# Clearing the region tails earlier and transposing a block ahead in an attention + mixture-of-experts + feed-forward kernel

## Chip, cores and metric

The kernel runs on one NeuronCore of a Trainium2 chip. The metric is the device time of one launch in microseconds (us), the median of several runs. Engines are TensorE (PE in the profile, PEld for its weight loads), VectorE (DVE), ScalarE (ACT), GpSimd (POOL) and SyncE (SP). SP issues most of the DMAs; a row with a q behind the engine's name (SPq, ACTq) is work of that engine's instruction sequencer: a register load, a branch, the issue of a DMA.

## What is computed

Three stages follow one another on 3072 tokens (4 sequences of 768) of width 384, all in float32.

```
for t in range(S):                                   # 1: gated linear attention, complex decay
    S_re, S_im = (ar*S_re - ai*S_im + k[t] (x) v[t], ar*S_im + ai*S_re)
    y[t] = q[t] . S_re
...
e_idx = argmax(x @ w_gate, axis=1)                   # 2: top-1 mixture of 8 experts
for e in range(E):
    mask = e_idx == e
    h = np.maximum(x[mask] @ w1[e], 0.0)
    out[mask] = gate_w[mask, None] * eom[mask, e, None] * (h @ w2[e])
...
h = x @ w_in                                         # 3: leaky feed-forward
return np.maximum(0.01 * h, h) @ w_out
```

## The kernel before

**Attention** (0 to about 290 us) works on 24 chunks of 128 tokens. Each finished row, its gate and its token number go from an SBUF ring to a DRAM table `x_sorted` (in the code `xs`): the table has one region per expert, and POOL scatters 128 rows of 386 floats with one indirect DMA (`scatter`, L563). The last two scatters belong to the last group of chunks.

**Tails.** The last block of a region is read as a full 128 rows, so the 128 rows behind each region's end must be zero. They are written from a constant tile `zeros`, one DMA of 128 x 386 floats per expert, as soon as DVE has written the ends (`ends_i`, semaphore `s_ends`). SP clears the tails of experts 0 and 1 (L1834 to L1837) and ACT those of experts 2 to 7 (L1997 to L2001). ACT does so only when the first block's tokens have landed (`s_xb`), and ahead of its first `relu`.

**The unused path.** Between attention and the expert stage DVE, ACT and PE each load a flag (L1352) and jump over a general attention path that these inputs don't need (the branches are L1389 on ACT, L1506 on DVE, L1601 on PE). After its jump ACT increments `s_moved` (L169), for which SP waits before it loads the first block.

**Experts** (about 293 to 569 us) work on blocks of 128 sorted rows, 29 of them here. The steps of block g:

- `load(g)` on SP: four DMAs that bring the block to the single buffer `x_q`, when `turn_tokens(g-1)` has emptied it (`s_tx`); `gates(g)`: one small DMA of the gates; `store(g)`: the block's result to `y_sorted`, when `result(g)` has made it. SP runs them in the order `load(g+3)`, `gates(g+2)`, `store(g)`.
- `turn_tokens(g)` on DVE: a 32 x 32 transpose from `x_q` to the PSUM bank `tx_bank` (L2025). `block_tokens(g)` on DVE: two instructions that split the bank into a leading and a trailing part in `x_tr` (L2031, L2033), when layer 1 of the block before is done with `x_tr`.
- `layer1(g)` on PE: 18 matmuls. `relu(g)` on ACT: two. `transpose_hidden(g)` on PE: 8. `leading(g)` on ACT and `trailing(g)` on DVE: two each, making `h_tr`. `layer2(g)` on PE: 24 matmuls. `result(g)` on DVE: one copy to `y_b` (L2046), when `store(g-1)` has landed.

PE runs `transpose_hidden(g)`, `layer1(g+1)`, `layer2(g)` in a loop over g. All instructions of an engine run in the order in which they are written; semaphores tie the engines together. Before block 0 DVE works out the table of blocks in small dependent steps: the first part (`s_rows`) gives the rows of each block, the second (`s_table`) the rest. PE fills its wait there with dummy transposes (`keep_warm`, L2203): 40, a wait on `s_rows`, then 22 more.

POOL meanwhile splits the next expert's weights (L1892, L1894) and requests the ones after it, a DMA of 1.5 MB (L1899), 14 times in the stage.

**Feed-forward** (from about 569 us) works on six windows of 512 tokens; PE runs `ff1` (L2168) and `ff2` (L2181) without a break.

Of the kernel before, what the change touches and what calls it, by code (L numbers as in the profile page):

```python
# [14 lines left out]
P = 128  # L15
# [8 lines left out]
E = 8  # L24
F1 = 1024
KT = W // P
Q = 4
# [33 lines left out]
def build(nc, in_a, in_qkv, moe_w, wg, wg_pairs, w_in, w_out, out):  # L61
# [3 lines left out]
    with ExitStack() as top:  # L65
# [72 lines left out]
        with ExitStack() as ctx:  # L138
            scan = attention(nc, ctx, sem, sb, in_a, in_qkv, wg_pairs, bank, ident, tri, stri, ones, wgp_sb, flag, stage, wm,
                             moe_w, xs, ledger, s_stage, s_split0, s_ends, s_flag, s_scat, s_fill, s_lg, s_lgc, s_k)  # L140
        with ExitStack() as ctx:
# [43 lines left out]
def attention(nc, ctx, sem, sb, in_a, in_qkv, wg_pairs, bank, ident, tri, stri, ones, wgp_sb, flag, stage, wm, moe_w, xs,  # L185
              ledger, s_stage, s_split0, s_ends, s_flag, s_scat, s_fill, s_lg, s_lgc, s_k):

# [443 lines left out]
    def scan_scalar(act):  # L631
# [3 lines left out]
        def squares(u):  # L635
            act.wait_ge(s_a[u % 3], 16 * (u // 3 + 1))
            need(act, s_turn, freed(u))
            act.activation(main[pair(u)][:, ucols(u)], a_in[pair(u)][:, 0, ucols(u)], ACT.Square).then_inc(s_sq, 1)
            act.activation(log_sq[pair(u)][:, ucols(u)], a_in[pair(u)][:, 1, ucols(u)], ACT.Square).then_inc(s_sq, 1)
# [91 lines left out]
        def gate_exps(g):  # L731
# [3 lines left out]
            act.activation(of_group(sel, g), of_group(sel, g), ACT.Exp, scale=-1.0).then_inc(s_ge, 1)  # L735

        squares(0)
        squares(1)
# [29 lines left out]
        for n in range(NCH + 1):  # L768
# [23 lines left out]
            else:  # L792
# [25 lines left out]
                if u is not None:  # L818
                    logs(u)

    def scan_vector(dve):
# [451 lines left out]
def attention_any(nc, sem, new, in_a, in_qkv, bank, ident, stri, ones, wg, flag, x_all, xs, ledger, s_flag, s_scat, s_fill, s_tail):  # L1273
# [68 lines left out]
    def enter(eng):  # L1342

        eng.sem_inc(s_enter, 1)
        eng.wait_ge(s_enter, 3)
        eng.wait_ge(s_fill, 48)
        for i in range(3):
            eng.wait_ge(s_scat[i], 16 * sum(size for _, size in GROUPS[i::3]))
# [365 lines left out]
def experts_then_feed_forward(nc, ctx, sem, sb, bank, ident, ids, stage, masks_at, wm, wbase, w_out_r, ys, moe_w, w_in,  # L1714
# [73 lines left out]
    def second_before_last(eng):  # L1788
        return at(eng, T_LAST, 2, N // P - 3, NBMAX - 3)
# [17 lines left out]
    def layers_sync(sp):  # L1807
# [10 lines left out]
        def gates(g):  # L1818
            need(sp, s_h, 2 * g)
            sp.dma_start(gate_b[:, :], xs[rows_of(g), W:W + 1], allow_slow_non_contiguous=True).then_inc(s_gate_in, 16)  # L1820
# [12 lines left out]
        sp.wait_ge(s_ends, 1)  # L1833
        for e in range(2):  # L1834

            row = sp.value_load(ends_i[0:1, e:e + 1], min_val=0, max_val=E * REG - P)
            sp.dma_start(xs[bass.ds(row, P), :], zeros[:, :]).then_inc(s_fill, 16)  # L1837
        for i in range(3):
            sp.wait_ge(s_scat[i], 16 * sum(size for _, size in GROUPS[i::3]))
        sp.wait_ge(s_moved, 1)  # L1840
        sp.wait_ge(s_fill, 48)
        load(0)
        gates(0)
        sp.wait_ge(s_rows, 1)
        load(1)
        sp.wait_ge(s_tail, 16 * (E - 2))
        load(2)
# [100 lines left out]
    def layers_scalar(act):  # L1948
# [47 lines left out]

        act.wait_ge(s_ends, 1)  # L1997
        act.wait_ge(s_xb, 16 * Q)
        for e in range(2, E):
            row = act.value_load(ends_i[0:1, e:e + 1], min_val=0, max_val=E * REG - P)  # L2000
            act.dma_start(xs[bass.ds(row, P), :], zeros[:, :]).then_inc(s_tail, 16)  # L2001
        relu(0)
# [18 lines left out]
    def layers_vector(dve, route_vector, sorted_slots):  # L2021
# [61 lines left out]
        dve.sem_inc(s_o, TW)  # L2083
        third = second_before_last(dve)
        trailing(0)
        turn_tokens(2)
        block_tokens(2)
        result(0)
        with dve.Fori(1, third + 1) as g:
            trailing(g)  # L2090
            turn_tokens(g + 2)
            block_tokens(g + 2)
            result(g)
        trailing(third + 1)
        dve.wait_ge(s_xl, third + 3)
# [13 lines left out]
    def layers_tensor(pe):  # L2109
# [98 lines left out]
        pe.wait_ge(s_rows, 1)  # L2208
        keep_warm(22)
        layer1(0)  # L2210
# [71 lines left out]
```

## Time and profile before

| | |
|---|---|
| median of 3 runs | 978.67 us |
| the three runs | 978.09, 978.67, 981.39 us |
| the profiled execution's own time | 978.09 us |
| its span, first to last instruction | 976.3 us |
| mean granted TensorE clock | 0.996 of full speed |
| attention | about 0 to 290 us |
| experts | about 290 to 569 us |
| feed-forward | about 569 to 976 us |

The profile is one execution. Times of rows are microseconds from the span's start. The row of an instruction group gives its start, its length, the engine and line, the tile written and the tile read, and in brackets how long the engine had been idle before it and what ended that. The chain of waits follows the work that ended last back from the end, step by step to what released it.

### The profile page before, as it was taken

Reading aid. Unit: us, or ns where it says so; the run is one execution under the profiler, and the core shown is the slowest. Engines: PE = TensorE matmul, PEld = TensorE weight load, DVE = VectorE, ACT = ScalarE, POOL = GpSimd, SP = SyncE. Lnnn points to the kernel's source line nnn. Section 1 sums busy time; section 2 is a strip of 40 time slices with the busy share of each in tenths; the row PEclk is TensorE's granted clock in tenths of the full one; section 3 lists DMA queues with packets and bytes.
Section 4 is the critical chain, followed back from the end, with each engine's and each line's share of the span. In section 5 each row is a group of like instructions: output and inputs, shape, how many; then the busy total and the mean of one; then the engine's idle time right before and its main releaser. Section 6 shows DMA issues by size and latency. Waiting matters only on the chain.

```text
span 976.3 us, 18188 instructions
## 1 busy us (share of the span) xinstructions
PE 940.3 (96%) x5904; PEld 836.7 (86%) x5905; DVE 438.7 (45%) x794; ACT 441.9 (45%) x742; POOL 510.1 (52%) x429
## 2 busy tenths in 40 slices
PE   5999999999879999999999999999999999999997
PEld 4777878887877989989999898999998999999997
DVE  5898898898846333433433432222222122222111
ACT  7999888997711222222222333333333333333322
POOL 4134656656464986767759923343243433423433
PEclk9999999999989999999999999999999999999999
DMA  3642363340153645335355520010010000000000
GB/s 121 205 139 83 113 238 99 101 137 2 64 183 94 205 133 167 113 105 169 113 169 169 130 57 17 9 41 17 9 49 17 29 21 17 33 1 1 33 1 32
DMA packets 74123, 83.89 MB, mean 86 GB/s; under 512 B 57653, under 2 KB 63305, under 8 KB 71497
## 3 DMA queue, kind: packets, MB, share of 16 engines
q1 hardware_dynamic: 67048, 47.20, 17.5%
q0 software_dynamic: 6144, 34.65, 10.2%
q10 hardware_dynamic: 864, 1.19, 0.3%
q8 instruction: 38, 0.62, 0.3%
q14 instruction: 29, 0.23, 0.1%
HBM read 65.59 MB, written 17.38 MB: 85 GB/s over the span
## 4 chain that ended last, share of the span: by engine, by line
PE 77%; ACT 10%; DVE 5%; issue 5%; DMA 1%; POOL 1%; ACTq 1%; SPq 0%; POOLq 0%; DVEq 0%
PE bank L2168 21%; PE bank L2181 20%; PE bank L2156 12%; PE bank L2131 12%; PE bank L2141 3%; PE bank L1098 2%; DVE neglog L850 1%; PE bank L1180 1%; PE bank L1138 1%; PE bank L1166 1%; PE bank L1140 1%; PE bank L1108 1%; PE bank L1121 1%; DVE neglog L857 1%; ACT log_sq L643 1%
## 5 line engine op out<-in xcount | busy, mean ns | idle before, releaser
L1922 POOL TENSOR_TENSOR act_r<-act_f,act_r 128x512 fp32r<-128x512 f32 x96 | 124.7, 1298 | 258.2 <-ACT act_r L1984 258.1
L2181 PE MATMUL bank<-w_out_r,act_r 128*128 128x384 f32 x1152 | 216.6, 336 | 0.3 <-POOL act_r L1922 0.3
L2168 PE MATMUL bank<-x,w_in_r 128*128 128x512 f32 x864 | 215.7, 394 | 0.0
L2181 PEld LDWEIGHTS bank<-w_out_r,act_r 128*128 128x128 f32 x1152 | 203.8, 188 | 9.1 <-POOL act_r L1922 0.6
L2063 DVE TENSOR_TENSOR act_f<-bank,small 128x512 f32<-128x512 f32 x96 | 66.5, 692 | 286.9 <-ACT small L1981 286.9
L2168 PEld LDWEIGHTS bank<-x,w_in_r 128*128 128x128 f32 x864 | 160.6, 187 | 30.1
L1981 ACT ACTIVATE small<-bank 128x512 f32<-128x512 f32 x96 | 57.5, 599 | 194.7 <-PE bank L2168 194.5
L2131 PE MATMUL bank<-wm,x_tr 128*128 (+1 forms) x522 | 129.1, 401 | 1.5 <-issue 1.0
L2156 PE MATMUL bank<-wm,h_tr 128*128 (+1 forms) x696 | 125.6, 336 | 0.0
L2156 PEld LDWEIGHTS bank<-wm,h_tr 128*128 128x128 f32 x696 | 121.5, 188 | 2.5
L2131 PEld LDWEIGHTS bank<-wm,x_tr 128*128 128x128 f32 x522 | 96.0, 188 | 23.3 <-issue 2.2
L1894 POOL TENSOR_TENSOR wm<-stage,wm 128x3072 fp32r<-128x3072 f32 x14 | 95.6, 6826 | 1.2
L1984 ACT ACTIVATE act_r<-act_f 128x512 fp32r<-128x512 f32 x96 | 60.7, 633 | 72.8 <-DVE act_f L2063 72.8
L1953 ACT ACTIVATE h<-bank,gate_b 128x512 f32<-128x512 f32 x58 | 36.8, 686 | 105.9 <-PE bank L2131 95.6
L1961 ACT ACTIVATE h_tr<-bank 128x512 fp32r<-128x512 f32 x58 | 31.7, 597 | 102.2 <-PE bank L2141 100.7
L1892 POOL TENSOR_SCALAR wm<-stage 128x3072 fp32r<-128x3072 f32 x14 | 39.0, 2783 | 43.0 <-PE bank L2131 17.4
L2046 DVE COPY y_b<-bank 128x384 f32<-128x384 f32 x29 | 16.2, 558 | 89.5 <-PE bank L2156 76.1
L1121 PE MATMUL bank<-q_t,k_t 96*128 96x128 f32 x384 | 54.3, 284 | 1.7 <-ACT q_t L698 1.2
L1138 PE MATMUL bank<-ident,qr 128*96 128x128 f32 x192 | 45.1, 275 | 5.6 <-DVE qr L913 5.5
L1121 PEld LDWEIGHTS bank<-q_t,k_t 96*128 96x128 f32 x384 | 46.7, 192 | 2.8 <-ACT q_t L698 2.1
L2040 DVE TENSOR_TENSOR h_tr<-bank,h_tr 128x512 fp32r<-128x512 f32 x58 | 37.4, 685 | 22.3 <-ACT h_tr L1961 22.3
L1140 PE MATMUL bank<-ident,kr 128*96 128x128 f32 x192 | 44.5, 272 | 0.0
(195 smaller groups left out, 1363.9 us busy)
## 6 DMA issues: line engine op xcount, KB each, us to landing
stage<-moe_w POOLq DMA_DIRECT2D x12, 1536.0 KB, 7.3
qkv_in<-in_qkv SPq DMA_DIRECT2D x24, 576.0 KB, 6.0
a_in<-in_a SPq DMA_DIRECT2D x11, 768.0 KB, 5.2
stage<-moe_w SPq DMA_DIRECT2D x4, 1536.0 KB, 7.1
x_q<-x_sorted SPq DMA_DIRECT2D x116, 48.0 KB, 1.9
y_sorted<-y_b SPq DMA_DIRECT2D x29, 192.0 KB, 1.9
xg<-y_sorted SPq DMA_DIRECT2D x96, 48.0 KB, 1.9
stage<-w_out POOLq DMA_DIRECT2D x2, 1536.0 KB, 7.0
```

The lines of the kernel that those rows point to most:

```text
L1121: last = pe.matmul(sc_bank[:, a * C:(a + 1) * C], k_t[h][:, a * C:(a + 1) * C], q_t[h][:, a * C:(a + 1) * C], start=True, stop=True)
L1138: pe.transpose(qt_bank[0:2 * D, a * C:(a + 1) * C], qr[n % 2][:, head, :, :].rearrange("p c d -> p (c d)"), ident[:, :])
L1140: last = pe.transpose(kt_bank[0:2 * D, a * C:(a + 1) * C], kr[n % 2][:, head, :, :].rearrange("p c d -> p (c d)"), ident[:, :])
L1894: pool.tensor_tensor(trail, half, lead.bitcast(F32), ALU.subtract).then_inc(s_wh, 1)
L1922: pool.tensor_tensor(a[:, 1, :], act_f[f % 2][:, :], a[:, 0, :].bitcast(F32), ALU.subtract).then_inc(s_gl, 1)
L1981: act.activation(small[f % 2][:, :], h_bank[f % 2][:, :], ACT.Copy, scale=0.01).then_inc(s_c, 1)
L1984: act.activation(act_r[f % 4][:, 0, :], act_f[f % 2][:, :], ACT.Copy).then_inc(s_gh, 1)
L2063: dve.tensor_tensor(act_f[f % 2][:, :], h_bank[f % 2][:, :], small[f % 2][:, :], ALU.max).then_inc(s_g, 1)
L2131: last = pe.matmul(hid_bank[j][:, :], x_tr[:, xp, t * P:(t + 1) * P], wmf[:, part_of(base, wp * WE + t * F1 + j * 512, 512)], start=(t == ...
L2156: last = pe.matmul(to_bank[:, 0:W], h_tr[:, hp, t * P:(t + 1) * P], wmf[:, part_of(base, wp * WE + t * W, W)], start=(t == 0 and n == 0), ...
L2168: last = pe.matmul(h_bank[f % 2][:, :], w_in_r[:, wp, t * F2 + f * P:t * F2 + (f + 1) * P], window_part(w, xp)[:, t, :], start=(t == 0 and ...
L2181: last = pe.matmul(o_bank[j][:, 0:W], a[:, ap, j * P:(j + 1) * P], w_out_r[:, wp, f * W:(f + 1) * W], start=(f == 0 and n == 0), stop=(f = ...
```

## The change

Three things change.

- **Tails.** SP clears the tails of experts 0 to 3, right after `s_ends` and ahead of its first `load`. ACT clears those of experts 4 to 7 at the end of its attention code (`clear_tails`), ahead of the flag and the jump. `load(0)` waits for tail 0 alone (`s_fill` 32 with the early fill in it), `load(1)` for all of the others (`s_tail`). ACT's six clears ahead of `relu(0)` are gone.
- **The DVE loop.** `turn_tokens` runs one block further ahead. Before: `trailing(g)`, `turn_tokens(g+2)`, `block_tokens(g+2)`, `result(g)`. Now: `trailing(g)`, `block_tokens(g+2)`, `turn_tokens(g+3)`, `result(g)`. Ahead of the loop `turn_tokens(2)` goes in front of `trailing(0)`.
- **PE** issues 28 dummy transposes behind `s_rows` in place of 22.

```diff
+        def clear_tails():
+            act.wait_ge(s_ends, 1)
+            for e in range(E // 2, E):
+                row = act.value_load(ends_i[0:1, e:e + 1], min_val=0, max_val=E * REG - P)
+                act.dma_start(xs[bass.ds(row, P), :], zeros[:, :]).then_inc(s_tail, 16)
...
                 if u is not None:
                     logs(u)
+        clear_tails()
...
         sp.wait_ge(s_ends, 1)
-        for e in range(2):
+        for e in range(E // 2):
 
             row = sp.value_load(ends_i[0:1, e:e + 1], min_val=0, max_val=E * REG - P)
-            sp.dma_start(xs[bass.ds(row, P), :], zeros[:, :]).then_inc(s_fill, 16)
+            sp.dma_start(xs[bass.ds(row, P), :], zeros[:, :]).then_inc(s_tail if e else s_fill, 16)
         for i in range(3):
             sp.wait_ge(s_scat[i], 16 * sum(size for _, size in GROUPS[i::3]))
         sp.wait_ge(s_moved, 1)
-        sp.wait_ge(s_fill, 48)
+        sp.wait_ge(s_fill, 32)
         load(0)
         gates(0)
+        sp.wait_ge(s_tail, 16 * (E - 1))
         sp.wait_ge(s_rows, 1)
         load(1)
-        sp.wait_ge(s_tail, 16 * (E - 2))
         load(2)
         gates(1)
...
-        act.wait_ge(s_ends, 1)
-        act.wait_ge(s_xb, 16 * Q)
-        for e in range(2, E):
-            row = act.value_load(ends_i[0:1, e:e + 1], min_val=0, max_val=E * REG - P)
-            act.dma_start(xs[bass.ds(row, P), :], zeros[:, :]).then_inc(s_tail, 16)
         relu(0)
...
         third = second_before_last(dve)
+        turn_tokens(2)
         trailing(0)
-        turn_tokens(2)
         block_tokens(2)
+        turn_tokens(3)
         result(0)
-        with dve.Fori(1, third + 1) as g:
+        with dve.Fori(1, third) as g:
             trailing(g)
-            turn_tokens(g + 2)
             block_tokens(g + 2)
+            turn_tokens(g + 3)
             result(g)
+        trailing(third)
+        block_tokens(third + 2)
+        result(third)
         trailing(third + 1)
...
         keep_warm(40)
         pe.wait_ge(s_rows, 1)
-        keep_warm(22)
+        keep_warm(28)
         layer1(0)
```

The order of two engines at these places. ACT, from its last activation of attention (L735) into the flag and the jump, before:

```order
L733 ACTIVATE soft<-soft 128x2x8
L735 ACTIVATE sel<-sel 128x2
L1352 TENSOR_LOAD flag
L1352 ISA x2
L1389 COMPARE_AND_BRANCH
```

and of the change, with the first of four clears (the same four rows follow three times more):

```order
L733 ACTIVATE soft<-soft 128x2x8
L735 ACTIVATE sel<-sel 128x2
L740 TENSOR_LOAD ends_i
L740 ISA x2
L741 ISA
L741 DMA x_sorted<-zeros 128x386
```

ACT now comes to the flag, the branch and the increment of `s_moved` behind four clears.

DVE, one turn of its loop over the blocks, from the two instructions of `trailing(g)` to `result(g)`, before (the name in brackets is the semaphore waited for):

```order
L2040 TENSOR_TENSOR h_tr<-bank,h_tr 128x512 [waits hidden_leading]
L2023 ISA
L2025 STREAM_TRANSPOSE bank<-x_q 128x4x3x32 [waits block_trailing,block_in]
L2029 REGISTER_ALU
L2031 CAST x_tr<-bank 128x384 [waits layer1_done,block_transposed]
L2033 TENSOR_TENSOR x_tr<-bank,x_tr 128x384 [waits block_leading]
L2044 REGISTER_ALU
L58 REGISTER_ALU [waits layer2_done]
L2046 COPY y_b<-bank 128x384 [waits block_stored]
```

and of the change:

```order
L2043 TENSOR_TENSOR h_tr<-bank,h_tr 128x512 [waits hidden_leading]
L2032 REGISTER_ALU
L58 REGISTER_ALU [waits block_transposed]
L2034 CAST x_tr<-bank 128x384 [waits layer1_done]
L2036 TENSOR_TENSOR x_tr<-bank,x_tr 128x384 [waits block_leading]
L2026 ISA
L2028 STREAM_TRANSPOSE bank<-x_q 128x4x3x32 [waits block_trailing,block_in]
L2047 REGISTER_ALU
L58 REGISTER_ALU [waits layer2_done]
L2049 COPY y_b<-bank 128x384 [waits block_stored]
```

The transpose of `x_q` has moved behind the split of the block before it, and `result` now stands behind a wait for a load (`block_in`).

## Rows read from the trace of the kernel before

**Rows 1.** Busy time by stretch: us, busy of each engine, PEclk, DMA share, GB/s

```profile
286.00:312.00 26.00, 23.52 (x144) 20.75 (x144) 14.76 (x45) 3.32 (x6) 10.46 (x18) 0.93 0.35 102
312.00:566.00 254.00, 254.00 (x1379) 230.58 (x1378) 97.23 (x170) 66.85 (x115) 199.86 (x75) 1.00 0.48 144
566.00:640.00 74.00, 74.00 (x372) 66.67 (x372) 17.54 (x28) 23.58 (x40) 22.04 (x17) 1.00 0.12 27
```

**Rows 2.** The chain of waits, 288 to 306 us: start, us, what

```profile
288.66 1.07 POOL x_sorted L563
289.73 0.30 issue
290.03 2.78 DMA x_sorted<-x_ring,pos
292.83 0.34 SPq L1815
...
294.17 1.87 DMA x_q<-x_sorted
...
302.12 0.34 ACTq L2001
...
302.56 0.70 ACT h L1953
303.25 0.04 issue
303.30 1.24 PE bank L2141 x8
304.53 1.00 issue
```

**Rows 3.** Instructions in order of time, all engines, 286 to 311 us

```profile
286.42 1.48 SPq L1837 DMA_DIRECT2D x_sorted<-zeros  x2
...
297.28 0.56 DVE L2033 TENSOR_TENSOR x_tr<-bank,x_tr 128x384 fp32r<-128x384 f32 x1
...
297.98 4.43 PE L2131 MATMUL bank<-wm,x_tr 128*128 128x512 f32 x18 [0.53 <-DVE x_tr L2033]
...
309.83 4.34 PE L2156 MATMUL bank<-wm,h_tr 128*128 128x384 f32 x24
```

**Rows 4.** The clears, sequencer times and landing: ACT's L2001, then SP's L1837

```profile
L2001 ACTq DMA_DIRECT2D x_sorted<-zeros x6: 338/352/405, 296.8 to 302.1; - x6
DMA to landing us min/median/max: 2.2/2.7/3.3
...
DMA to landing us min/median/max: 1.9/2.1/2.2
```

**Rows 5.** The flag and the jump on ACT and on DVE

```profile
L1352 ACTq TENSOR_LOAD <-flag x1: 487/487/487, 285.8 to 285.8; - x1
...
L169 ACTq EVENT_SEMAPHORE  x1: 17/17/17, 287.0 to 287.0; - x1
...
L1506 DVEq COMPARE_BRANCH  x1: 72/72/72, 288.7 to 288.7; - x1
...
291.62 0.20 DVE L1659 TENSOR_TENSOR held<-ends,region 128x8 f32<-128x8 f32 x1 [3.75 <-issue]
```

**Rows 6.** Busy time by stretch, columns as in rows 1

```profile
287.00:289.00 2.00, 2.00 (x12) 2.00 (x11) 0.17 (x1) 0.00 (x0) 0.86 (x4) 0.50 0.56 200
290.00:292.00 2.00, 2.00 (x21) 2.00 (x19) 0.34 (x2) 0.00 (x0) 1.87 (x9) 1.00 0.51 184
```

**Rows 7.** Landing of the block loads L1815, issued 297 to 299.3, then 292 to 294.5

```profile
DMA to landing us min/median/max: 2.2/2.9/3.2
...
DMA to landing us min/median/max: 1.8/1.9/2.0
```

**Rows 8.** The dummy transposes of PE, L2205

```profile
L2205 PE MATMUL bank<-ident,zeros x62: 272/273/328, 290.4 to 297.2; 128*128 128x128 f32 x62
```

**Rows 9.** Instructions in order of time, the expert loop around its longest store

```profile
380.64 0.37 SPq L1825 DMA_DIRECT2D y_sorted<-y_b  x1
...
383.30 1.95 SPq L1815 DMA_DIRECT2D x_q<-x_sorted  x4
...
390.42 0.56 DVE L2046 COPY y_b<-bank 128x384 f32<-128x384 f32 x1 [4.97 <-DMA y_sorted<-y_b]
390.90 1.28 DVE L2040 TENSOR_TENSOR h_tr<-bank,h_tr 128x512 fp32r<-128x512 f32 x2
...
393.29 2.94 PE L2156 MATMUL bank<-wm,h_tr 128*128 x16
```

**Rows 10.** Landing of the loads issued 383 to 385 us, L1815

```profile
DMA to landing us min/median/max: 5.7/5.8/6.4
```

More of the change, by code:

```diff
@@ L139, in build @@
             scan = attention(nc, ctx, sem, sb, in_a, in_qkv, wg_pairs, bank, ident, tri, stri, ones, wgp_sb, flag, stage, wm,
-                             moe_w, xs, ledger, s_stage, s_split0, s_ends, s_flag, s_scat, s_fill, s_lg, s_lgc, s_k)
+                             moe_w, xs, ledger, s_stage, s_split0, s_ends, s_flag, s_scat, s_fill, s_tail, s_lg, s_lgc, s_k)
         with ExitStack() as ctx:
@@ L185, in attention @@
 def attention(nc, ctx, sem, sb, in_a, in_qkv, wg_pairs, bank, ident, tri, stri, ones, wgp_sb, flag, stage, wm, moe_w, xs,
-              ledger, s_stage, s_split0, s_ends, s_flag, s_scat, s_fill, s_lg, s_lgc, s_k):
+              ledger, s_stage, s_split0, s_ends, s_flag, s_scat, s_fill, s_tail, s_lg, s_lgc, s_k):
     qt_bank, kt_bank, kh_bank, qh_bank = bank[0], bank[1], bank[2], bank[3]
@@ L1345, in enter @@
         eng.wait_ge(s_enter, 3)
-        eng.wait_ge(s_fill, 48)
+        eng.wait_ge(s_fill, 32)
+        eng.wait_ge(s_tail, 16 * (E - 1))
         for i in range(3):
```

## The prediction

> **What bounds the kernel now.** I read the busy times by stretch first, since the three edits all lie between 286 and 566 us and the question is where TensorE is ever without work there. From 312 to 566 us PE is busy for 254.00 of 254.00 us, from 566 to 640 us for 74.00 of 74.00, and from 286 to 312 us for 23.52 of 26.00 [rows 1]. So there are 2.5 us of idle PE time that any of these edits could remove, all of it at the seam between attention and the experts, and the expert loop has none. The dummy transposes count as busy in that row, so the seam has to be read from the chain of waits. It runs [rows 2]: the last scatter of POOL is issued at 290.03 and lands 2.78 us later, at 292.81; SP issues `load(0)` from 292.83; the last of its four parts, issued at 294.17, lands 1.87 us later; DVE transposes and splits it until 297.84; `layer1(0)` runs on PE from 297.98 [rows 3]; then comes ACT with its last clear, `relu(0)` at 302.56, the eight transposes at 303.30, 1.00 us of PE's sequencer, and `layer1(1)`.
>
> **The sum, part by part.** I add up against the profiled execution: 978.09 us, a span of 976.3 and 1.8 around it. It was the lowest of three runs; the median is 0.58 higher.
>
> *Clears gone ahead of `relu(0)`.* They look dear: six issues between 296.8 and 302.1 [rows 4], about 1.06 us each with the register loads, and ACT's last one, from 302.12 for 0.34 us, stands in the chain right ahead of `relu(0)` [rows 2]. But `relu(0)` needs `layer1(0)` too, and that ran from 297.98 for 4.43 us, until 302.41 [rows 3]. ACT was free at 302.46. With the clears gone `relu(0)` starts some 0.1 us earlier at most, since PE is late next. Value: **-0.1 us**.
>
> *`load(1)` and `load(2)` without clears beside them.* The parts of `load(1)`, issued while the clears were on their way, took 2.9 us where those of `load(0)` took 1.9 [rows 7]. That gives back up to 1 us of landing, but block 1 is not needed before `layer1(1)` at 305.53, which follows the sequencer's 1.00 us behind the transposes, and block 2 not before `layer2(0)` at 309.83 has ended [rows 2, 3]. Value: 0.
>
> *Clears put earlier.* ACT's four now stand between its last activation and the flag. ACT read the flag from 285.8 and incremented `s_moved` at 287.0, 1.2 us for flag, branch and increment [rows 5]. Now: 285.8 + 4 x 1.06 + 1.2 = 291.2. SP waits for `s_moved` only in front of `load(0)`, and that waits for the scatter until 292.81 [rows 2]: 1.6 us to spare, cost 0. SP's own four: two took 1.48 us from 286.42 [rows 3], so four, at 1.1 us each, are issued by 290.2, again ahead of 292.81; cost 0 on SP.
>
> The price is on the DMA engines. From 287 to 289, with the two clears of SP on their way, the share was 0.56 over 2 us, so one clear is 0.56 us of all sixteen engines; from 290 to 292, with the two last scatters, it was 0.51, so a scatter is about 0.5 us [rows 6]. Now eight clears are issued from 286.1 to 290.2: 8 x 0.56 = 4.5 us, with the first scatter 5.0 us of work, where the engines have 4.0 us from 287 until the last scatter's data starts, at about 291. About 1.0 us of other work is then still queued, and the last scatter's 0.5 us has to share with it. Its delay lies between 0 (all its packets go first) and 1.0 us (it ends with the last clear). The nearest row for a transfer that meets clears is that of `load(1)`, +1.0 us at the median, +0.3 at the least [rows 7]. I take 0.7 us, since this queue is short-lived and the scatter has not the whole of it ahead. `load(0)` has no cover: it is the chain. Value: **+0.7 us** (0 to +1.0).
>
> The page "DMA: Bandwidth & Descriptors" of the Trainium skill, section on queues, rings and completion order, says that each DMA engine goes round the queues that have work, a packet at a time. By that rule the scatter queue would share evenly with SP's and ACT's clears of about 0.5 us each, all three would end together, and the term would be its upper end, +1.0 us. No row here shows three queues at once.
>
> *Six more dummy transposes.* The 62 start from 290.4 to 297.2 [rows 8], 61 steps of 0.11 us. Six more are 0.67 us, so they end at about 297.98, just when `layer1(0)` started before [rows 3]. If x_tr comes 0.7 us late they are hidden; if it does not they still cost 0.0 to 0.1. Only if `s_rows` comes late do they stand in the way, since 28 of them, 3.1 us, are behind it. Value: 0.
>
> *The DVE loop.* It makes a load land earlier on paper, but no PE time waits for one there [rows 1]. What it adds is a wait: `result(g)`, and behind it `trailing(g+1)`, which PE needs for `layer2(g+1)`, are queued on DVE behind `turn_tokens(g+3)`, which waits for `load(g+3)`. The load itself goes out sooner: its buffer is free a block earlier, so SP issues it right behind `store(g-1)` and no longer behind `turn_tokens(g+2)`. The tightest place before is at 390 us: the store issued at 380.64 was in the way of a weights load and landed at about 390.4, `result` started 4.97 us late at 390.42, `trailing` at 390.90, and PE still began `layer2` at 393.29 without idling [rows 9]. The first half of `trailing` (0.64 us) ended at 391.55, 1.7 us early. The loads issued from 383.30 then, the last at about 384.9, took 5.7 to 6.4 us [rows 9, 10], so they were in by 390.4 as well. Issued 1.7 us earlier they should land no later. Then `turn_tokens` adds its own 0.58 us ahead of `result`, and 1.1 us remain. The first `trailing`, behind `turn_tokens(2)` now, has room of the same kind: `load(2)` no longer waits for clears. Value: 0, covered by those 1.1 us.
>
> Sum: -0.1 + 0.7 = **+0.6 us**. 978.09 + 0.6 = 978.7 for an execution like the profiled one, and 978.67 + 0.6 = **979.3 us** for the median.
>
> **The rivals.**
>
> *A. Nothing is delayed.* The scatter's data gets through in time, and the seam gains 0.1 us: 978.6. For it: the clears of ACT start at once, at 286.1, when the engines are idle. Against it: the sum of the shares.
>
> *B. ACT's jump stalls, and `load(0)` waits for `s_moved`.* DVE's branch at 288.7 was followed by its next instruction only at 291.62, 2.9 us later, while ACT's 1.2 us from flag to increment hold no such gap [rows 5]. If ACT's branch costs another 2.9 us now, `s_moved` comes at 291.2 + 2.9 = 294.1, 1.3 us behind the scatter; with the -0.1: 979.9. For it: same kind of jump, and busy DMA engines. Against it: ACT jumps over the same stretch of code as before. The page "Runtime: NRT & Kernel Launch" of the Trainium skill, section on instruction fetch mechanics, says that a taken branch whose target isn't among the two blocks of instructions at hand forces a fetch. By that rule, the shift of ACT's code by four clears could put the target on the other side of a block's edge, and rival B would follow. The trace has one case of each kind, DVE's and ACT's.
>
> *C. The loop stalls PE: slower.* The mechanism is the new place of `result` behind the load. In the case of rows 9 the last part of the load would now be issued at 383.2; `turn_tokens`, `result` and the first half of `trailing` take 0.58 + 0.56 + 0.64 = 1.8 us and must be done by 393.3, so it decides from a landing of 8.3 us on. The store in the same place needed 9.8 us (380.64 to 390.4) [rows 9]. If the loads took 9.8 us too, PE would wait 1.5 us. There are 14 weights loads; at one in five meeting it, 3 x 1.5 = 4.5 us, and with the +0.6: 983.8. Against it: the loads beside that store needed 6.4 at most, and both ended together, with the weights load [rows 10].
>
> *D. Something in the trace of one execution misleads by more than 0.3%.* For a gain this would need more idle PE time than the 2.5 us of rows 1.
>
> **How the numbers follow.** A measurement of this kernel can tell about 0.3% (2.9 us) from no change. Forecast (the scatter late by 0.3 to 1.0 us, 978.9 to 979.6): 0.55. A: 0.25. B: 0.11. C: 0.05. D: 0.02 faster, 0.02 slower. The likeliest gives 979.3. The range starts at rival A less its scatter, 978.6 - 0.6 = 978.0, and ends at B with the spread by which medians of this kernel's runs may differ (the third run was 2.7 us above the second, of which I take 1.1): 981.0. C and D, and some of B's upper end, stay out. Faster: 0.02. Slower: 0.05 + 0.02 = 0.07. Same: 0.91.
>
> **What would show it.** The last scatter lands at 293.1 to 293.8 in place of 292.81, with a DMA share above 0.9 from 288 to 292, and `load(0)` is issued right behind it: forecast. It lands by 292.9: A. `load(0)` is released by ACT's increment: B. Idle PE time between 312 and 566 us, ahead of `layer2`, released by `h_tr`: C. `layer1(0)` starts 0.3 to 1.0 us later than 297.98, and `relu(0)` within 0.1 us of its end. The forecast is wrong if PE's busy time from 312 to 566 falls short of the stretch, or if the seam, from the last scatter's issue to the start of `layer1(1)`, 15.5 us before, differs by more than 1.5 us.

## The result, and the profile after

The changed kernel takes 987.96 us (median of 6 runs, 984.39 to 990.56). The kernel before, timed beside it, takes 980.92 us (6 runs, 978.09 to 983.14). The ratio is 1.0070 with a 95% interval of 1.0043 to 1.0098 (here and below the ratio is an estimate of its own, which need not be the quotient of the two medians): slower by 0.7%, about 7 us, where +0.6 us was forecast. The prediction was wrong.

The profiled execution of the changed kernel took 985.73 us, 7.64 more than the one of before. First the busy times by stretch, as in [rows 1] (the first stretch begins 2 us earlier here): us, busy time of PE, PEld, DVE, ACT and POOL, granted clock, DMA share, GB/s.

```profile
284.00:312.00 28.00, 23.58 (x142) 20.67 (x143) 13.20 (x45) 2.56 (x5) 9.20 (x22) 0.90 0.34 94
312.00:566.00 254.00, 251.00 (x1350) 227.53 (x1350) 94.27 (x166) 64.50 (x110) 200.77 (x75) 0.99 0.46 141
```

The expert loop, without a hole before, has 3.0 us of idle PE time, and its clock is no longer 1.00. The seam has to be read from the chain of waits, as in [rows 2]; each row is start us, us, what.

```profile
287.85 1.07 POOL x_sorted L563
288.92 0.30 issue
289.22 5.80 DMA x_sorted<-x_ring,pos
295.04 0.34 SPq L1823
...
296.38 1.90 DMA x_q<-x_sorted
298.30 0.60 DVE bank L2028
```

The last scatter is issued 0.8 us earlier than before and takes 5.80 us to land in place of 2.78. All behind it is as before: SP goes on 0.02 us after the landing, the load takes 1.90 us (1.87). The same stretch in order of time (start, duration, instruction, in brackets the idle time ahead of it and what ended that) shows that PE now stands there:

```profile
300.23 4.43 PE L2138 MATMUL bank<-wm,x_tr 128*128 128x512 f32 x18 [2.50 <-DVE x_tr L2036]
...
304.76 1.26 ACT L1961 ACTIVATE h<-bank,gate_b 128x512 f32<-128x512 f32 x2 [19.60 <-PE bank L2138]
...
307.75 4.46 PE L2138 MATMUL bank<-wm,x_tr 128*128 x18 [1.01 <-issue]
```

From the last scatter's issue to `layer1(1)` it is 307.75 - 289.22 = 18.5 us, where it was 15.5. This is the first 3.0 us.

What the DMA engines did meanwhile, us by us, in the columns of the first view:

```profile
287.00:288.00 1.00, 1.00 (x7) 1.00 (x6) 0.06 (x1) 0.00 (x0) 0.15 (x1) 0.50 0.97 344
...
291.00:292.00 1.00, 1.00 (x12) 1.00 (x11) 0.66 (x3) 0.00 (x0) 0.15 (x1) 1.00 1.08 343
292.00:293.00 1.00, 1.00 (x12) 1.00 (x11) 0.90 (x4) 0.00 (x0) 0.00 (x0) 1.00 0.48 133
293.00:294.00 1.00, 1.00 (x12) 1.00 (x10) 0.90 (x3) 0.00 (x0) 0.00 (x0) 1.00 0.13 38
294.00:295.00 1.00, 1.00 (x10) 0.85 (x9) 0.35 (x2) 0.00 (x0) 0.00 (x0) 1.00 0.03 12
```

They are full from 287 to 292 and through with most of it at 292.5, as the sum of shares had it. But the scatter's landing is seen only at 295.02, after 2.5 us at shares of 0.13 and 0.03. The DMA view tells what was under way in this time. From 292.5 to 295.2 us, by queue (q0 is POOL's, q10 ACT's, q1 SP's): packets, MB, share of all sixteen engines.

```profile
q0 software_dynamic: 16, 0.04, 4.4%
q10 hardware_dynamic: 16, 0.02, 2.3%
q1 hardware_dynamic: 9, 0.01, 1.7%
```

So the clears were not through either. In the trace's packet records the last packet of SP's clears ends at 293.51 us, that of ACT's at 294.01 and that of the scatter at 294.51, and from 293.5 on the packets of these three queues follow one another, none beside another but for one of 4 bytes. One engine of sixteen is 0.06 of the share: by this estimate a single engine was 1 to 2 us behind the others, and the scatter lands with the last of them. Which engine it was, and why it was behind, the records don't say. `e1_clears` below shows the same end. Its last clear, which ACT issued at 295.1, landed 4.8 us later, at 299.9, and the last scatter, issued at 294.49, at 300.19.

Then the hole in the loop. The waits between 312 and 570 us (who, for what, us in total, times, longest):

```profile
DVE bank L2028 <- DMA x_q<-x_sorted: 80.3, 25, 9.2
...
PE bank L2163 <- DVE h_tr L2043: 3.0, 1, 3.0
```

Before, PE never waited for `h_tr` there, and from 300 us on DVE hardly for `x_q`; the row of before in the same view:

```profile
DVE bank L2025 <- DMA x_q<-x_sorted: 2.9, 2, 2.5
```

The place of the hole in the changed kernel, in order of time:

```profile
346.91 0.59 DVE L2028 STREAM_TRANSPOSE bank<-x_q 128x384 f32<-128x384 f32 x1 [5.74 <-DMA x_q<-x_sorted]
347.41 0.53 DVE L2049 COPY y_b<-bank 128x384 f32<-128x384 f32 x1
...
348.78 0.37 SPq L1833 DMA_DIRECT2D y_sorted<-y_b  x1
...
349.78 0.59 POOL L1907 DMA_DIRECT2D stage<-moe_w  x1 [0.30 <-POOL wm L1902]
350.61 2.12 SPq L1823 DMA_DIRECT2D x_q<-x_sorted  x4
...
357.91 1.08 ACT L1969 ACTIVATE h_tr<-bank 128x512 fp32r<-128x512 f32 x2 [7.38 <-remote]
359.59 0.59 DVE L2028 STREAM_TRANSPOSE bank<-x_q 128x384 f32<-128x384 f32 x1 [9.17 <-DMA x_q<-x_sorted]
...
360.55 1.27 DVE L2043 TENSOR_TENSOR h_tr<-bank,h_tr 128x512 fp32r<-128x512 f32 x2
...
361.48 5.85 PE L2163 MATMUL bank<-wm,h_tr 128*128 x24 [3.00 <-DVE h_tr L2043]
```

The load's last part, in the chain of waits:

```profile
352.34 7.22 DMA x_q<-x_sorted
```

It reads as a circuit: transpose of `x_q`, `result`, store, and only behind the store, in SP's order, the next load, for which the next transpose waits. From the transpose (346.91) to the last of the load's four issues (352.34 in the chain of waits) these fixed parts take 5.4 us of a block's 9.25 us. Here the load left just behind a load of weights (349.78, 1.5 MB) and took 7.22 us. From the transpose to `layer2` it is another 1.9 us, and PE was free at 358.48: as far as this circuit goes, a landing of up to 4.2 us would have been in time. (ACT's leading half at 357.91 is late as well, which is taken up under `e13_load_first`.) The cost is 3.0 us of idle PE, and 5.85 us for matmuls that otherwise take 4.33, since the granted clock fell (the third number from the right in these stretches):

```profile
360.00:361.00 1.00, 0.00 (x0) 0.00 (x0) 1.00 (x3) 1.00 (x2) 1.00 (x1) 1.00 0.00 0
361.00:362.00 1.00, 0.52 (x2) 0.53 (x3) 1.00 (x3) 0.23 (x1) 1.00 (x1) 0.58 0.00 0
...
363.00:364.00 1.00, 1.00 (x5) 1.00 (x4) 0.00 (x0) 0.00 (x0) 1.00 (x1) 0.50 0.00 0
```

A wait of 0.69 us ahead of `layer2` at 572.32 follows later. The account of the 7.64 us: attention 0.8 us shorter (the scatter's issue), seam +3.0, the hole +4.5, from there to the feed-forward part +0.95: 7.65.

### The profile page after: what moved, and what is told of

Read it like the earlier page. It is cut to its first block, busy times and chain, and to the rows that moved or that the text cites. A ratio compares the mean times of both kernels' runs of the same rounds, so it can differ in the third digit from the quotient of the medians.

```text
span 984.0 us, 18194 instructions
## 1 busy us (share of the span) xinstructions
PE 943.6 (96%) x5910; PEld 839.4 (85%) x5911; DVE 437.6 (44%) x794; ACT 441.6 (45%) x742; POOL 509.2 (52%) x429
## 4 chain that ended last, share of the span: by engine, by line
PE 67%; ACT 10%; DVE 6%; DMA 6%; issue 6%; SPq 4%; POOL 1%; DVEq 0%; POOLq 0%; ACTq 0%
PE bank L2175 20%; PE bank L2188 20%; PE bank L2163 8%; PE bank L2138 7%; DMA x_q<-x_sorted 5%; PE bank L1105 2%; PE bank L2148 2%; SPq L1823 1%; DVE neglog L857 1%; PE bank L1187 1%; PE bank L1145 1%; PE bank L1173 1%; PE bank L1147 1%; PE bank L1115 1%; PE bank L1128 1%
## 5 line engine op out<-in xcount | busy, mean ns | idle before, releaser
L2028 DVE STREAM_TRANSPOSE bank<-x_q 128x384 f32<-128x384 f32 x29 | 17.2, 593 | 87.6 <-DMA x_q<-x_sorted 87.5
```

## Experiments

Three theories stood to be told apart. **The scatter** waits for the clears that are now ahead of it. **The loop**: the new order on DVE closes the circuit above. **Clock or dummies**: the 28 dummies, or the idle time, do it by TensorE's clock. "Only" below means on top of the kernel before; "the clears" are all parts of the change's diff that clear the tails and wait for it.

### Each part alone

`e1_clears`: the clears only, 22 dummies. 

> The kernel before with the move of the clears alone (SP clears tails 0 to 3, ACT 4 to 7 ahead of its flag; the DVE loop and 22 dummy transposes as before). Theory S (the seam): eight clears beside the last two scatters fill the DMA engines, and load(0) starts 3.0 us later behind the last scatter's issue (5.8 us where it was 2.8). It expects a time 2.5 to 3.5 us above before, no PE idle time between 312 and 566 us, and a landing of the last scatter above 5 us. Theory P (phase): the seam only shifts the loads against the weights loads and the cost would vanish or vary; it expects 0 to 1 us or a spread with no sign. Theory L (the loop alone costs the time): within 1 us of before.

`e2_loop`: DVE's new order only (its part of the diff, unchanged). 

> The kernel before with the new order of the DVE loop alone (clears and dummy transposes as before). Theory L: the loop's new order closes a circuit, load(g+3) -> turn_tokens(g+3) -> result(g) -> store(g) -> load(g+4), and a load that meets a weights load holds up trailing(g+1) and PE: 3 to 6 us above before, PE idle ahead of layer2 in at least one block, DVE waits on x_q above 50 us in all. A part of this, about 1.5 us, comes from trailing(0) behind turn_tokens(2), since load(2) here still waits for ACT's late clears. Theory P (the loop is harmless by itself, and stalled only because the seam had shifted it against the weights loads): below 2 us, all of it at the first block.

`e3_warm`: the dummies only.

```diff
-        keep_warm(22)
+        keep_warm(28)
         layer1(0)
```

> The kernel before with 28 dummy transposes behind s_rows in place of 22, nothing else. All theories: within 0.5 us of before; layer1(0) starts within 0.1 us of where it did.

`e5_no_loop`: clears and 28 dummies, DVE's loop as before. 

> The changed kernel with the DVE loop of before: early clears and 28 dummy transposes. Theory S+L (the seam costs 3.0 us by the late scatter, the loop 4.3 us by itself, and the clock gate adds to the first where PE idles long ahead of layer1(0)): 2.3 to 3 us above before at the same mean granted clock, and below the run with 22 dummy transposes, since the idle stretch ahead of layer1(0) is 0.5 to 0.7 us shorter and PE falls to its lower clock there less often. Rival (28 transposes do nothing for the clock): the same time and the same mean clock (0.990) as with 22.

| kernel | median us (runs) | before beside it | ratio, 95% |
|---|---|---|---|
| e1_clears | 985.20 (10) | 979.44 (31) | 1.0049, 1.0030 to 1.0069 |
| e2_loop | 984.74 (10) | 979.44 (31) | 1.0047, 1.0028 to 1.0066 |
| e3_warm | 979.34 (10) | 979.44 (31) | 0.9999, 0.9984 to 1.0014 |
| e5_no_loop | 979.77 (5) | 977.33 (15) | 1.0038, 1.0021 to 1.0055 |

Both the clears and the loop cost time on their own; the dummies alone change nothing that these runs can tell. The loop alone has the same signs (DVE waits 82.7 us for `x_q` in 28 cases) and its hole in the same block, though ACT's leading half was there on time, at 352.66 us. The two waits of PE for `h_tr` in `e2_loop`, from the order of time:

```profile
310.36 4.40 PE L2160 MATMUL bank<-wm,h_tr 128*128 128x384 f32 x24 [0.69 <-DVE h_tr L2040]
...
359.12 4.44 PE L2160 MATMUL bank<-wm,h_tr 128*128 x24 [2.29 <-DVE h_tr L2040]
```

In the profiled execution the clears alone cost twice. In `e1_clears` the scatter lands after 5.70 us, and PE is idle for 2.8 us. Its `layer1(0)`, in order of time:

```profile
305.44 7.24 PE L2134 MATMUL bank<-wm,x_tr 128*128 128x512 f32 x18 [2.80 <-DVE x_tr L2036]
```

And the same time in stretches of 1 us, with the granted clock third from the right:

```profile
304.00:305.00 1.00, 0.00 (x0) 0.00 (x0) 0.93 (x3) 0.00 (x0) 0.00 (x0) 0.90 0.00 0
305.00:306.00 1.00, 0.56 (x1) 0.50 (x2) 0.93 (x4) 0.00 (x0) 0.00 (x0) 0.50 0.08 13
```

`layer1(0)` takes 7.24 us at the lower of the clock's two levels (0.50 of 2.4 GHz is 1.2) in place of 4.43. The profiled executions of the changed kernel, after 2.5 us of idle time at the same place, and of `e10_ids_apart` below, after 2.94, kept their clock there (4.43 us).

Not all of this execution's time is the clears', though. It took 987.93 us, 9.8 more than the profiled one of before, and its last scatter is issued 4.5 us later (294.49 for 290.03). Its granted clock was 0.50 from 278 to 290 us, where before has 0.72, and the first clear was issued only at 290.89. The profiled execution of `e7_short_weights` below has the same in attention (0.51, the scatter at 295.10) and a `layer1(0)` of 4.43 us. To `e1_clears` the seam adds 5.6 us: 2.9 by the scatter, 2.8 by `layer1(0)`.

Its executions span 980.9 us (mean clock 0.994) to 987.93 (0.985). Seven of the ten have a mean clock of 0.990 or less, of before on the same chip 4 of 31, and of `e5_no_loop` on another none of 5. The two kernels, whose scatters differ by 0.5 us, stand 5.8 and 2.4 us above before, and beyond the scatter's part the difference goes with the low clocks. Whether a clock was low ahead of `layer1(0)` or in attention is seen in the profiled execution alone. That the six dummies are what sets the two kernels apart is therefore not shown.

### How much of the clears the scatter waits for

`e8_half_early`: clears and 28 dummies, old loop, but only SP's four clears early; ACT's four stand where ACT's six stood before.

```diff
-        clear_tails()
...
+        act.wait_ge(s_xb, 16 * Q)
+        for e in range(E // 2, E):
...
```

> As the run without the loop change, but only SP's four clears are early; ACT's four stand behind the landing of load(0) as before, and load(2) waits for them. Theory S (the bytes of the early clears hold up the last scatter; the engines were full at eight): the last scatter lands 2.8 to 4 us after its issue, and the time is within 1 us of before. Rival (any clear beyond the first two, or the wait for ACT, makes the scatter late): 5 us or more, and 2 to 3 us above before.

`e12_sp_spread`: the kernel before, but SP issues all clears, one early, one behind the first gates, six behind `load(1)`.

```diff
-        for e in range(2):
+        for e in range(1):
...
         load(1)
+        for e in range(2, E):
+            row = sp.value_load(ends_i[0:1, e:e + 1], ...)
+            sp.dma_start(xs[bass.ds(row, P), :], zeros[:, :]).then_inc(s_tail, 16)
```

> The kernel before with SP alone clearing the tails: tail 0 ahead of load(0), tail 1 behind gates(0), tails 2 to 7 behind load(1); ACT clears none; 22 dummy transposes, the old DVE loop. One clear beside the last scatters in place of two. Theory S (each early clear costs the last scatter about 0.5 us of DMA time): the scatter lands 0.2 to 0.5 us earlier than in before (2.8 us from its issue), relu(0) starts 0.1 us earlier, the time is 0 to 0.7 us below before, which three rounds can't tell from no change. Rival (SP's loads get late behind its own clears): 1 to 2 us above before, with PE idle ahead of layer1(1) or layer1(2).

| early clears | last scatter's landing, us | kernels |
|---|---|---|
| 1 | 2.60 | e12_sp_spread |
| 2 | 2.72 to 2.79 | before, e2_loop, e3_warm |
| 4 | 4.08 | e8_half_early |
| 8 | 5.24 to 6.24 | the changed kernel and all with its clears |

`e8_half_early` takes 979.86 us (10 runs) against 977.33, ratio 1.0022 (1.0001 to 1.0043), 2.5 us above before where within 1 us was expected. Each clear beyond the second adds about (5.8 - 2.78) / 6 = 0.5 us, near the 0.56 us of all engines that one clear is [rows 6]. So the scatter waits for practically all the clears around it, though it is in another queue. By the packets above, the last 1 to 2 of the 3 us pass while one or two engines work off what they have of all three queues.

`e12_sp_spread` has the shortest scatter and is still slower than before: 982.41 us (4 runs) against 978.79, ratio 1.0045 (1.0028 to 1.0063), as its rival had it. SP now comes late with the gates and the next loads; in order of time, behind the first block:

```profile
314.69 1.24 PE L2142 MATMUL bank<-ident,h 128*128 128x128 f32 x8 [1.19 <-ACT h L1959]
317.11 6.00 PE L2132 MATMUL bank<-wm,x_tr 128*128 x18 [1.19 <-issue]
```

The second row is slow by the clock: it was granted at 0.50 from 318 to 320 us, after two gaps of only 1.19 us, and `layer1(2)` took 6.00 us for 4.45. The kernel gave back about 0.2 us of scatter and lost more behind it. The place of the clears before, on ACT behind the first load, is better than any tried here.

`e11_warm_through`: the clears with 50 dummies (keep_warm(50) ahead of `layer1(0)`), old loop. 

> The changed kernel with the DVE loop of before and 50 dummy transposes behind s_rows in place of 28, so that PE has work right up to layer1(0). Theory G (the idle stretch ahead of layer1(0), about 3 us with 22, 2.3 with 28, lets PE's clock fall in some executions, and layer1(0) then takes 6.8 us where it takes 4.4): no execution below 0.992 of mean clock, layer1(0) 4.4 us, the median 2.5 to 3 us above before, no execution above 983. Rival (the low clocks come from attention and have nothing to do with the stretch): the clocks spread as in before, and as with 28.

980.75 us (7 runs) against 978.79, ratio 1.0027 (1.0010 to 1.0045). The scatter takes 5.76 us, PE is idle for 0.88 us in place of 2.8, `layer1(0)` takes 4.43, and no execution's mean clock is under 0.994 (before beside it has 0.992 to 0.997). More dummies leave the scatter's part as it is. That they take the clock's part away fits these seven executions, and is not shown, since before had no low clock on this chip either.

### What the loop's price hangs on

`e4_result_first`: the changed kernel, `result(g)` ahead of `turn_tokens(g+3)` (and `result(0)` ahead of `turn_tokens(3)`).

```diff
             block_tokens(g + 2)
-            turn_tokens(g + 3)
             result(g)
+            turn_tokens(g + 3)
```

> The changed kernel with result(g) ahead of turn_tokens(g+3) in the DVE loop (and result(0) ahead of turn_tokens(3)); the clears and the dummy transposes as changed. The store no longer hangs on the load, but trailing(g+1) is still queued behind the wait for load(g+3). If the circuit through the store is what stalls PE, the loop's part goes (4 to 5 us) and the seam's 3 us stay: 983 to 985. If it is only the wait ahead of trailing, the time stays at that of the changed kernel, 986 to 989.

`e13_load_first`: the changed kernel, DVE's new order kept, but SP issues each load ahead of the store of the block four behind it.

```diff
-        store(0)
         with sp.Fori(1, third) as g:
             load(g + 3)
+            store(g - 1)
             gates(g + 2)
-            store(g)
+        store(third - 1)
```

> The changed kernel with one edit on SP: in the loop over the blocks the load of block g+4 is issued ahead of the store of block g, not behind it (order load, store, gates in a turn). VectorE's new order stays as it is. Circuit theory (a load waits behind the store of the result, the result behind the transpose, the transpose behind the load, so that a load has only about 4 us from its last issue until TensorE stands): the load now leaves right behind the transpose of the block before it, about 3 us earlier in a turn, and near 350 us it leaves ahead of the load of the weights. The waits of VectorE for x_q fall from about 80 us in all to under 15, TensorE waits for no h_tr ahead of layer 2, and the time comes to about 980 us, as with the result put first: what is left is the scatter's delay of 3 us at the seam. Weights theory (the load of x_q is slow whenever the weights move, wherever it is issued): x_q waits of 5 us and more remain, TensorE still loses 3 us or more ahead of layer 2, 985 us or more. A third cause, ScalarE's late leading half by 3 to 4 us in the block near 355 us: if it is there for a reason of its own, TensorE still waits about 1 us there, 981 to 982 us.

Each opens the circuit at another place. `e4_result_first` takes 980.79 us (10 runs) against 979.44, ratio 1.0025 (1.0006 to 1.0043), less than the 983 to 985 expected; `e13_load_first` 981.00 us (10 runs) against 977.20, ratio 1.0035 (1.0023 to 1.0048). DVE's long waits for `x_q` are gone. The view of the waits, of `e4_result_first`:

```profile
DVE bank L2028 <- DMA x_q<-x_sorted: 9.2, 9, 2.9
```

The same view of `e13_load_first`, with all that PE waited for ahead of `layer2`:

```profile
DVE bank L2028 <- DMA x_q<-x_sorted: 7.1, 3, 3.0
...
PE bank L2163 <- issue: 0.3, 1, 0.3
```

What is left to both is the scatter (5.79 and 5.93 us). The second also answers a question that the changed kernel's trace had left open, ACT's leading half there at 357.91, some 3.6 us late without having waited for PE. `e13_load_first` has 2.9 us of this lateness in the same block, with the load in time:

```profile
352.91 2.41 SPq L1823 DMA_DIRECT2D x_q<-x_sorted  x4
...
357.20 1.09 ACT L1969 ACTIVATE h_tr<-bank 128x512 fp32r<-128x512 f32 x2 [6.65 <-issue]
357.83 1.29 DVE L2043 TENSOR_TENSOR h_tr<-bank,h_tr 128x512 fp32r<-128x512 f32 x2 [3.73 <-issue]
358.79 4.43 PE L2163 MATMUL bank<-wm,h_tr 128*128 x24 [0.29 <-issue]
```

There it costs PE 0.29 us. From ACT's start to `layer2` it is 1.59 us here. In the changed kernel ACT's start at 357.91 would by that have let `layer2` begin at 359.50, 1.0 us after PE was free (an estimate from these rows), so of its 3.0 us of idle time the load alone answers for 2.0, and ACT would have left 1.0 of it standing. In `e2_loop`, with ACT on time, the load alone made 2.29 us.

`e7_short_weights`: the changed kernel, but each load of expert weights inside the loop brings 64 columns instead of all, so experts after the first compute with mostly stale weights. This asks whether the loads must meet the weights.

```diff
-                pool.dma_start(half, lots[lot + 1][:, i * WE:(i + 1) * WE]).then_inc(s_more[i], 16)
+                pool.dma_start(half[:, 0:64], lots[lot + 1][:, i * WE:i * WE + 64]).then_inc(s_more[i], 16)
```

> The changed kernel with POOL's sixteen weights loads of the expert stage cut from 1.5 MB to 64 columns each (32 KB); what is multiplied is then mostly the first experts' weights, the work on every engine is the same. Theory L (the loads of x_q come late because weights loads fill the DMA engines, and the late load stalls PE through result and store): no PE idle time ahead of layer2, DVE waits on x_q down from 88 us to below 40, x_q landing 2 us throughout, and a time of before + 3 us (the seam alone), 982 to 983. Rival (the new DVE order stalls PE without any help from the DMA engines): 986 to 988, as the changed kernel.

981.48 us (6 runs) against 977.33, ratio 1.0039 (1.0025 to 1.0053), about the scatter's part and a little more; DVE's waits for `x_q` are 33.0 us in 28 cases, the longest 3.9, and PE waits for no `h_tr`. The circuit alone makes DVE wait 1.2 us a block, which is hidden; it takes the weights to make a wait that isn't.

`e10_ids_apart`: the changed kernel, POOL's scatters of sorted token numbers (L1911) ahead of the expert's split, so that they no longer follow a load of weights at once. `e9_changed_again` is the changed kernel as it is, for the same chip.

```diff
+            if 2 <= e < 2 + B:
+                sort_ids(range((e - 2) * NCH // B, (e - 1) * NCH // B))
             for i in range(2):
                 split(e, i, wm[:, e % 2, i, :], wm[:, e % 2, 2 + i, :], done)
-            if 2 <= e < 2 + B:
-                sort_ids(range((e - 2) * NCH // B, (e - 1) * NCH // B))
```

> The changed kernel with POOL's six small indirect DMAs per expert (sorted_ids) put ahead of that expert's weight split, so that they no longer follow a weights load at once. In the changed kernel PE's one stall in the loop (3.0 us ahead of layer2 near 361 us, and slower matmuls in it) lies where a weights load, the first six of these DMAs and a load of x_q meet. Theory M (the meeting of all three makes the load of x_q take 7 to 9 us): the stall is gone or below 1 us and the time 3 to 4.5 us below the changed kernel, 982 to 983.5. Rival W (the weights load alone does it): a stall of 2 us or more stays, and the time is that of the changed kernel, 986 to 987.

> The changed kernel as it is, beside the others on one chip. All theories: 6 to 8 us above before; the time of an execution falls with its mean granted clock by about 0.75 us per 0.001.

`e10_ids_apart` 985.39 us (4 runs), ratio 1.0073 (1.0052 to 1.0094); `e9_changed_again` 986.52 us (4 runs), ratio 1.0093 (1.0076 to 1.0110). The waits in `e10_ids_apart`:

```profile
DVE bank L2028 <- DMA x_q<-x_sorted: 73.3, 25, 6.7
...
PE bank L2163 <- DVE h_tr L2043: 3.4, 4, 1.4
```

And in `e9_changed_again`:

```profile
DVE bank L2028 <- DMA x_q<-x_sorted: 77.6, 27, 9.3
PE bank L2163 <- DVE h_tr L2043: 3.8, 2, 3.1
```

The repeat has the hole in the same block (361.20 us, 3.09), and `layer2` behind it took 7.16 us in place of 5.85. With the small scatters elsewhere the one long hole is gone, but four short ones (0.34, 1.39, 1.13 and 0.56 us) add up to 3.4 us. Three of the four stand behind a late leading half of ACT. The third of them, in `e10_ids_apart`:

```profile
397.41 1.08 ACT L1969 ACTIVATE h_tr<-bank 128x512 fp32r<-128x512 f32 x2 [7.49 <-remote]
...
399.00 4.43 PE L2163 MATMUL bank<-wm,h_tr 128*128 x24 [1.13 <-DVE h_tr L2043]
```

From ACT's start to `layer2` it is 1.59 us, as in `e13_load_first`, and at 340.47 it is too. The load's transposes had begun 0.9 and 1.4 us ahead of ACT in these two, so it is ACT's lateness, and not the load's landing, that sets them. Ahead of 369.86 both were late: the transposes began at 367.97, 1.89 us before `layer2` as in the changed kernel, and ACT at 368.15. So neither expectation for this run held, and it doesn't tell what part the small scatters have. ACT's lateness, by 2.7 to 3.9 us against its usual start 1.07 us behind the start of PE's transposes, occurs in this kernel three times, in the changed one, its repeat and `e13_load_first` once each, and in no profiled execution of the others. Its cause is open.

Executions with the same mean clock of 0.996 fit the account: before 976.57 to 978.28 us (18 executions with the profiled one's 978.09, the middle 977.1), `e4_result_first` 979.95 to 980.27, `e2_loop` 981.31 and 982.05, the changed kernel 984.39. The scatter's 3.1 us and the loop's 4.6, each from the middles of these, add up to 7.7 us, and 977.1 + 7.7 = 984.8. The groups are small, and a mean clock doesn't say where it was lost: the repeat has 986.32 us at 0.997, and `e11_warm_through`, with the scatter's part alone, one execution of 984.09 at 0.996.

## Why the prediction was wrong

*The clears put earlier, +0.7 us (0 to +1.0)*: the mechanism was right and the size wrong; it measured +3.0. The work, 8 x 0.56 us and two scatters, came out as reckoned (the engines were through with most of it at about 292.5). The step that failed is the size of the upper bound, "1.0 us (it ends with the last clear)". It does end with the last clear (299.9 and 300.19 in `e1_clears`), but the last clear ends well after the time by which the shares have the work done: the landing came 2.5 us after 292.5, at shares of 0.13 and 0.03, while one or two engines still had packets of all three queues. The mistake in method was to take both bounds from shares, which are means over sixteen engines. No row showed a scatter behind clears, and without one the upper bound should have been the whole of the clears' work, 4.5 us. The Trainium skill, "DMA: Bandwidth & Descriptors", section on queues, rings and completion order, has each engine go round its queues a packet at a time, by which the prediction drew the same +1.0. The trace agrees that the three end nearly together (293.51, 294.01 and 294.51), but the delay was +3.0 us: 0.5 us for each clear beyond the second.

*"Six more dummy transposes": 0.* Right for the dummies (`e3_warm`: 0.9999). Not seen was what idle time ahead of `layer1(0)` can do to the clock. With the scatter's 3 us, PE stood for 1.8 to 2.9 us there in the kernels with eight early clears and 22 or 28 dummies, and in one of the profiled executions, that of `e1_clears`, the next matmuls ran at half clock.

*The DVE loop, 0*: this was the largest error, +4.5 us in the hole and +0.95 behind it. The prediction named the wait behind which `result` is queued, as rival C, and gave it 0.05. Two steps failed. "Issued 1.7 us earlier they should land no later": the load was not issued earlier. The prediction let it go "right behind `store(g-1)`" but did not follow `store(g-1)` back to `result(g-1)` and that to the transpose, a circuit of 5.4 us of fixed parts in 9.25. In the block at 350 us the load went out at 350.61 to 352.34, 4.4 us later than its twin of before at 346.25 (2.2 of them the later start of the whole block), and the twin had left ahead of the weights. And so "it decides from a landing of 8.3 us on" was wrong too: in this block it decides from 4.2 us. Landings of 5.7 to 6.4 us stood in [rows 10]. Rows of the tightest place before are no bound when the change moves the issue itself.

*Rival C's price*, 3 x 1.5 = 4.5 us, agrees with the hole by chance: it was one hole of 3.0 us, of which ACT's lateness would have left 1.0, with 1.5 us for the clock behind it, not three. What was held against it, that "the loads beside that store needed 6.4 at most", counted only against the 8.3 us.

*ACT's clears gone ahead of `relu(0)`, -0.1*: right. `relu(0)` starts 4.53 us after `layer1(0)`, 4.58 before.

*`load(1)` and `load(2)`: 0*: right; `layer1(1)` still waits for the sequencer's 1.0 us.

*Rival B, ACT's jump*: not the case. The waits of SP near 290 us:

```profile
SPq L1823 <- DMA x_sorted<-x_ring,pos: 3.3, 1, 3.3
SPq L1848 <- ACTq L169: 2.1, 1, 2.1
```

ACT's increment came at 291.6, against 291.2 in the prediction, with no stall at its jump; SP waited 3.3 us more for the scatter. By the Trainium skill's page "Runtime: NRT & Kernel Launch", section on instruction fetch mechanics, ACT's shifted jump could have forced a fetch; this trace shows none there. *Rival A* fell with the scatter.

*The signs to look for* did their work: the share above 0.9 from 288 to 292 was seen in part (0.89 in the first us), the scatter at 295.02 in place of 293.1 to 293.8, and "the forecast is wrong if PE's busy time from 312 to 566 falls short of the stretch" and a seam that differs from 15.5 us by more than 1.5 both came true.

What stays open: why one DMA engine ends so long after the others at the seam, why ACT is 2.7 to 3.9 us late in one to three blocks of four of these kernels, and why the clock fell behind the idle 2.8 us of `e1_clears` and two gaps of 1.19 us in `e12_sp_spread` and not behind the 2.94 of `e10_ids_apart`.

## What to carry to other kernels

When an order is changed, write down the full circuit through all in-order queues (here load, transpose, result, store, load), add its fixed parts, and compare the landing it leaves with the slowest landing in the trace, not with the landing at today's time of issue. A DMA on the critical path is to be costed as waiting for all the bytes issued around it, in whatever queue, until a run shows otherwise, and a mean share over all engines doesn't show the one that ends last. Dummy work that keeps TensorE busy can at best keep the clock up; it does not shorten the gap it fills.

## What the runs showed of the hardware

- A scatter of 128 rows in POOL's queue landed in 2.6, 2.7, 4.1 and 5.2 to 6.2 us with 1, 2, 4 and 8 clears (128 x 386 floats each) of SP and ACT issued around it: 0.5 us for each beyond the second. I had expected 1.0 us in all. With eight, in the changed kernel, its last 2.5 us passed at a mean share of 0.13 and less of the sixteen engines.
- A 48 KB load issued behind a load of weights of 1.5 MB landed in 7.2 us; issued just ahead of one, in 1.8 us.
- Idle gaps of PE of 2.8, 3.0 and 3.1 us were followed by a granted clock of 0.50: from about 305 us in `e1_clears` (a layer of 7.24 us for 4.43), in the changed kernel from 361.5 us (5.85 for 4.33) and in its repeat (7.16 for 4.33). Two gaps of 1.19 us with 1.24 us of transposes between them were followed by it, too, in `e12_sp_spread` (6.00 for 4.45). During the gaps of 2.8 and 3.0 us the rows still show 1.00 or 0.90. Gaps of 2.94 us in `e10_ids_apart` and of 2.29 in `e2_loop` were not followed by it.
